# First batch of a fused attention and channel-mixing kernel: ScalarE's DMA issues, weight squares and weight scaling moved to later steps, and value products of two heads put ahead of a score block on TensorE

## The reference

```
q_d, k_d, v_d = means over groups of 4 tokens           # 144 pooled tokens
out_up    = repeat(softmax(q_d k_d^T / 8) v_d, 4)       # pooled attention
out_local = softmax(masked(q k^T / 8)) v                # mask: |i - j| < 4
x   = heads joined: out_up + out_local                  # [4, 576, 512]
u   = x + real(fft over tokens, then over features)
un  = (u - mean) / sqrt(var + 1e-6)
x2  = u + relu(un @ w_ch1) @ w_ch2                      # 512 -> 2048 -> 512
gate = sigmoid(causal convolution of x2 with 5 taps per channel)
out = (gate * (x2 @ w_val)) @ w_out
```

## Time and profile before

| | us |
|---|---|
| median of 3 runs | 789.04 |
| the three runs | 782.66, 790.0, 789.04 |
| the profiled execution, whole | 786.93 |
| its span, first to last instruction | 785.1 |
| TensorE busy | 721.6 (92%) |
| VectorE busy | 387.2 (49%) |
| ScalarE busy | 193.7 (25%) |
| GpSimd busy | 152.2 (19%) |

### The profile page before, as it was taken

The page is one execution under the profiler, slowest core; times in us unless marked ns, Lnnn a source line. Parts: engine busy times, 40 slices in busy tenths (PEclk is TensorE's granted clock), DMA queues, the critical chain, the costliest instruction groups (busy, mean ns, idle before and its releaser), DMA issues.

```text
span 785.1 us, 15614 instructions
## 1 busy us (share of the span) xinstructions
PE 721.6 (92%) x5960; PEld 538.5 (69%) x5960; DVE 387.2 (49%) x925; ACT 193.7 (25%) x417; POOL 152.2 (19%) x130
## 2 busy tenths in 40 slices
PE   2569959999999998999999998999999999999998
PEld 1445547876767776876767776877667677777776
DVE  4447585554535943533544872543553861113452
ACT  1527522222211122322212122222212131111201
POOL 8001777971102221001101311000101300000000
PEclk9999859999999999999999999999999999999999
DMA  9994227032001045022001136022000000000001
GB/s 258 287 247 111 84 91 192 14 72 64 1 1 59 27 130 120 1 65 65 7 1 31 39 85 180 1 58 65 14 1 1 1 31 31 1 1 1 2 15 46
DMA packets 42096, 49.07 MB, mean 62 GB/s; under 512 B 4784, under 2 KB 35568, under 8 KB 40944
## 3 DMA queue, kind: packets, MB, share of 16 engines
q1 hardware_dynamic: 32608, 31.06, 15.7%
q10 hardware_dynamic: 9424, 17.06, 7.0%
HBM read 43.38 MB, written 4.72 MB: 61 GB/s over the span
## 4 chain that ended last, share of the span: by engine, by line
PE 78%; DVE 8%; DMA 5%; issue 3%; POOL 3%; SPq 1%; ACT 1%; ACTq 0%; DVEq 0%; POOLq 0%
PE P L561 23%; PE Y L578 22%; PE P L691 4%; PE Y L680 4%; PE A L587 4%; PE Y L691 4%; DMA kl<-qk_win 3%; DVE prob_or_un L1100 2%; PE A L548 2%; PE A L541 2%; PE A L531 2%; PE A L641 1%; PE A L484 1%; PE A L630 1%; PE P L541 1%
## 5 line engine op out<-in xcount | busy, mean ns | idle before, releaser
L578 PE MATMUL Y<-hT,w 128*128 128x288 f16 x1536 | 215.5, 286 | 5.8 <-DVE xT L1156 5.8
L561 PE MATMUL P<-unT,w_wv 128*128 128x288 f16 x1536 | 212.1, 290 | 6.4 <-issue 5.0
L1135 DVE SCALAR_TENSOR_TENSOR hT<-P,hT 128x288 f16<-128x288 f32 x128 | 58.5, 457 | 268.9 <-ACT hT L815 268.9
L561 PEld LDWEIGHTS P<-unT,w_wv 128*128 128x128 f16 x1536 | 150.1, 99 | 51.7 <-issue 12.0
L578 PEld LDWEIGHTS Y<-hT,w 128*128 128x128 f16 x1536 | 144.9, 98 | 49.8 <-DVE xT L1156 6.1
L815 ACT ACTIVATE hT<-P 128x288 f16<-128x288 f32 x128 | 52.5, 411 | 218.3 <-PE P L561 216.8
L1171 DVE SCALAR_TENSOR_TENSOR gate<-xT,cw,gate 128x288 f32<-128x288 f32 x128 | 68.6, 536 | 4.5
L786 ACT ACTIVATE prob_or_un<-prob_or_un 73x288 f32<-73x288 f32 (+1 forms) x52 | 23.3, 448 | 95.9 <-DVE prob_or_un L1008 92.1
L1306 POOL MEMSET x<- 1x512 f32 x4 | 2.1, 516 | 212.5 <-ACT x L804 212.5
L317 POOL TENSOR_TENSOR x<-x,fb 128x256 f32<-128x256 f32 (+1 forms) x12 | 12.1, 1005 | 107.9 <-DVE fb L1076 107.9
L691 PE MATMUL P<-shared,wo 128*128 128x288 f32 x128 | 32.1, 409 | 0.7 <-DVE shared L1181 0.5
(11 more groups left out here) (162 smaller groups left out, 843.0 us busy)
## 6 DMA issues: line engine op xcount, KB each, us to landing
kl<-qk_win SPq DMA_DIRECT2D x38, 140.0 KB, 5.5
ql<-qk_win SPq DMA_DIRECT2D x19, 256.0 KB, 3.9
vl<-v_win SPq DMA_DIRECT2D x72, 65.0 KB
pair_or_folded<-qk_pool SPq DMA_DIRECT2D x8, 580.0 KB, 5.9
pair_or_spectrum<-qk_pool SPq DMA_DIRECT2D x8, 580.0 KB, 6.5
out<-ot ACTq DMA_DIRECT2D x32, 144.0 KB, 1.8
w_wv<-w_ch ACTq DMA_DIRECT2D x4, 1024.0 KB, 13.3
w<-w_ch ACTq DMA_DIRECT2D x4, 1024.0 KB, 12.6
```

Source lines behind the costliest of these rows:

```text
L561: last = mm(P[s % 2][:, 0:HN], w1s(k, f, wt), unT[:, ut, k, ha * HN:(ha + 1) * HN], start=k == 0 and wt + ut == 0, stop=k == KD - 1 and wt ...
L578: last = mm(Y[d][:, 0:HN], w2s(f, d, wt), hT[s % 3][:, ht, :], start=f == 0 and wt + ht == 0, stop=f == KF - 1 and wt == 1)
L1135: nc.vector.scalar_tensor_tensor(out=hT[s % 3][:, 1, :], in0=P[s % 2][:, 0:HN], scalar=0.0, in1=hT[s % 3][:, 0, :], op0=ALU.max, op1=ALU.s ...
```

## The change

Five tables of the first step get other numbers, `W1_AT` goes from 9 to 10, and on TensorE the scores of local unit 9 move behind the value products of heads 6 and 7. The w1 loads go two steps later, the first two w2 loads one or two, the sixteen issues of the value windows, in groups of four, from steps 2 to 5 to steps 8 to 11, the w1 squares up to two steps later, the w1 halves one step later. The numbers of instructions are the same.

```diff
--- before.py
+++ after.py
@@ -241,13 +241,13 @@
 
         POOLING = {3: 2, 5: 3}
         POOLING_FIRST = {1: 1, 3: 2, 5: 3}
-        WEIGHT_LOADS = {2: [0], 3: [1], 4: [2], 5: [3], 7: [4], 8: [5], 11: [8, 6], 12: [7]}
-        SQUARES = {5: [0, 1], 6: [2, 3], 7: [4, 5], 8: [6, 7], 13: [8], 14: [9, 10], 15: [11], 16: [12, 13]}
-        W1_HIGH = {10: [0, 1], 11: [2, 3], 12: [4], 13: [5], 14: [6], 15: [7]}
-        FIRST_VALUES = {2: (2, 0), 3: (2, 1), 4: (3, 0), 5: (3, 1)}
-        W1_LOW = {11: [0, 1], 12: [2, 3], 13: [4], 14: [5], 15: [6], 16: [7]}
+        WEIGHT_LOADS = {4: [0], 5: [1], 6: [2], 7: [3], 8: [4], 9: [5], 11: [8, 6], 12: [7]}
+        SQUARES = {7: [0, 1], 8: [2, 3, 4, 5], 9: [6, 7], 14: [8, 9], 15: [10], 16: [11, 12, 13]}
+        W1_HIGH = {11: [0, 1], 12: [2, 3], 13: [4, 5], 14: [6], 15: [7]}
+        FIRST_VALUES = {8: (2, 0), 9: (2, 1), 10: (3, 0), 11: (3, 1)}
+        W1_LOW = {12: [0, 1], 13: [2, 3], 14: [4, 5], 15: [6], 16: [7]}
         SEQ_AT, FEAT_AT = 24, 29
-        W1_AT = 9
+        W1_AT = 10
         TILE_ORDER = [0, 3, 1, 4, 2, 5]
         FOLD_AFTER = [2, 3, 4]
         CONSTS = 6 * 16
@@ -706,10 +706,10 @@
                             pair_scores(b, s)
                         elif UD <= s < NU and s != UD + 1:
                             unit_scores(b, s)
-                            if s == UD:
-                                unit_scores(b, s + 1)
                         for u in done:
                             unit_av(b, u)
+                        if s == UD:
+                            unit_scores(b, s + 1)
                 for s in range(SLOTS + LAG_DOWN if m is not None else 0):
                     down = s >= LAG_DOWN
                     if s < SLOTS:
```

## The result

In 20 runs each the changed kernel has a median of 791.49 us (787.3 to 797.09), the kernel before 786.3 (782.66 to 790.19). The ratio is 1.0062, with a 95% interval of 1.0042 to 1.0081: about 4.9 us slower. The forecast was 789.8, within 1% of no change. Its 2.9 us stood against an execution of 786.93, close to the median of the 20 runs, so 2.9 forecast stands against 4.9 measured (3.3 to 6.4 by the interval).

The account below looks back on a forecast made before the run. It took the first batch's attention to be bound by a chain: a key-window DMA, TensorE, then GpSimd. 1.8 at unit 8's transposes plus 1.1 late made 2.9, so 786.93 + 2.9 = 789.8 us, range 783 to 797.

Parts of the forecast that it names:

- Up to head 6, a gain: ScalarE's opening: fewer issues and squares ahead of copies 1 and 3; exponential 6 moves from 33.76 to 31.2.
- Relief of the queues: DMA queues in the opening: without ScalarE's value windows, the second key window lands at 36 to 39 instead of 44.3.
- Copies of heads 5 to 7: ScalarE: value issues at 2.88 a group put copies 5, 6, 7 at 36.1, 43.55, 48.3; copy 7 is 6.4 late.
- The bounds, 1.8 and 5.1 a group: ScalarE's value issues, taken at 2.88 a group: the cheap bound gives 786.6; the dear one adds 6.8 over three groups.
- The swap repairs part of the damage: TensorE, products before unit 9's scores: alone worth up to 3.6; with the issues, unit 8's transposes come 1.8 late.
- The fourth group "takes nothing": ScalarE before unit 8's copy: the fourth value issue ends at worst at 58.4, needed at 58.3; counted as nothing.
- The late stage, +1.1: Step 13 on: second low half and later squares delay unit 11's copy, folds and w2 sum, 1.1 more.
- The sum at the w2 sum: TensorE's w2 sum before the loop: 1.8 + 1.1 = 2.9 us late, at 90.5 instead of 87.58.
- Rival 1: Opening: value issues cost ScalarE next to nothing and TensorE uses the earlier window; 781.7 to 784.4, chance 0.14.
- Rival 2: ScalarE's value issues stall at 5.1 a group, adding 6.8 before copy 7; at least 798.2, chance 0.08.
- The loop unchanged: Channel-mixing loop after about 116 us: shifted by about 3 and otherwise unchanged.

Follow-up runs that it names:

- experiment 3: Changed kernel with the sixteen value issues back in steps 2 to 5, all else changed: 789.36 us, ratio 1.0047 to the kernel before.
- experiment 2: Changed kernel without the swap, scores of unit 9 directly behind those of unit 8 on TensorE: 791.85 us, ratio 1.0041 to the kernel before.
- 6: Kernel before with the TensorE swap and W1_AT 10 instead of 9, tables as before: 790.01 us, ratio 1.0017.
- experiment 4: Changed kernel with one w1 high and one low half a step from step 13 on, instead of two: 790.01 us, ratio 1.0051 to the kernel before.
- experiment 5: Kernel before with only the changed late stage (w1 halves, and squares from step 14 on): 789.74 us, ratio 1.0012.
- experiment 7: Kernel before with the swap, W1_AT 10, DFT tables one step later and the w2 loads behind them two steps later: 785.89 us, ratio 0.9961.
- experiment 8: Kernel before with swap, W1_AT 11, changed w1 loads, later tables, single halves, value issues in ScalarE's gaps: 786.72 us, ratio 0.9988.
- experiment 9: Changed kernel with value issues back in steps 2 to 5, single w1 halves, later DFT tables and w2 loads: 784.15 us, ratio 0.9952 to kernel before.
- experiment 10: Changed kernel with only the DFT tables and the w2 loads behind them later: 791.54 us, ratio 1.0058 to the kernel before.
- experiment 1: Kernel before with only the TensorE swap (products of heads 6 and 7 ahead of unit 9's scores): 790.24 us, ratio 1.0051.

## Why the prediction was right, point by point

The range, the sign and the class held; the sum was 2 us short, just outside the measured interval of 3.3 to 6.4. The range, 783 to 797, took in a gain as well as a loss, so that it held says little; the milestones say more. Taking the trace of after against the steps:

- **Up to head 6, a gain**: right. Exponential 6 at 30.74 (31.2 forecast).
- **Relief of the queues**: the direction was right, the size too small. I put the key window of unit 9 at 36 to 39; its two DMAs were issued from 13.17 on and took about 11 to 13 us, so it landed near 26. "They trade packet for packet" held, 505 to 508 and 99 to 95 now, and so did the end of the first w1 loads at about 22. What I left out is the stretch behind it: with almost nothing on ScalarE's queue SyncE's moved 943 packets in 3 us, against 508 in 7 before.
- **Copies of heads 5 to 7**: the step right, its term too small. 36.30 (36.1 forecast), 44.53 (43.55) and 49.71 (48.3). The groups of four issues took 3.46, 3.41 and 3.23 us from first to last (32.26 to 35.72 is the first), not the 2.88 of the earlier trace rows. The excess, 0.58 + 0.53 + 0.35 = 1.5, is about the miss at unit 8's transposes: +3.2 instead of +1.8. The trace of the kernel before already had such a group, its first, which I did not take:

```profile
8.25 3.47 ACTq L875 DMA_DIRECT2D unT<-v_win  x4
```

The bounds, 1.8 and 5.1 a group, took it in. This is **the largest mis-sized term of the sum**, with the clock below. Experiment 3 shows the cause: with the issues back, the transposes come at 49.0.
- **The swap repairs part of the damage**: wrong, though the sum it stands in held (from unit 9's scores to unit 8's transposes 4.1 us, 51.20 to 55.27, against 7.6 before). Without the swap unit 9's scores were not late at all (40.88 in experiment 2). Experiments 2 and 6 show that with the later scale it is worth 3.6 where TensorE waits for the window of unit 9, and that it costs 0.9 where head 7's copy is late.
- **The fourth group "takes nothing"**: off by 0.6 (+3.8 at unit 8's product, +3.2 at its transposes). I had counted the 2.86 of the value issues, not the three issues of step 11 behind them, ahead of the same copy: two of tables, 0.45 and 0.47 (56.82, 57.30), and a w2 load that took 1.73 (57.80) instead of the 0.38 of the earlier trace rows.
- **The late stage, +1.1**: the mechanism is in the trace: two low halves make the fold late, TensorE stood 1.08 for it (0.25 with single halves, experiment 4). Its price in time is not shown: experiment 5 has +0.9 for this part alone, with an interval from -0.6 to +2.4. Nor are two halves the only thing that makes this wait: experiments 7 and 8, with single ones, waited 1.47 and 0.82. What I had not in the sum is TensorE's level. The 2.54 us for unit 11's copy only used up what two units at the upper level had won (unit 10's transposes at 68.42 against 64.64, +3.8; unit 11's product at 77.39 against 73.65, +3.7). But after it the level was the lower one, granted 0.50 from 78 to 90, and the first twelve matmuls of the DFT took 2.29 + 2.30 + 2.08 instead of what the kernel before shows:

```profile
80.29 3.96 PE L587 MATMUL A<-sdft,pair_or_folded 128*128 128x289 f32 x8
84.18 1.33 PE L587 MATMUL P<-sdft,pair_or_folded 128*1 128x289 f32 x4
```

6.67 against 5.29 is 1.4 us. From unit 12's product (+3.7) to the w2 sum (+6.2) the loss is 2.5 = 1.08 + 1.4. That the stand of 2.54 brought the lower level is not shown: the same twelve took 6.3, 6.5 and 6.3 us in experiments 3, 8 and 9, which had neither that stand nor an upper stretch before it, and 4.8 in experiment 5. So the kernel before may have been fast by chance here; why the level rises sooner in one trace than in another is open.
- **The sum at the w2 sum**: 2.9 + 1.4 (issues) + 0.6 (fourth group) + 1.4 (level) = 6.3; the trace has 6.2. Over many runs it is 4.9; both traces are of single executions, in which the place of the upper level and of the late window varies.
- **Rival 1 (relief)**: its premise, cheap issues, is refuted: 2.9 to 3.5 us a group. (The estimate of 0.2 a group, worked out from the 50 ns of dispatch in the Trainium skill, DMA: Bandwidth & Descriptors, Anatomy of one DMA, does not hold here; that section describes DMAs issued by GpSimd, not by ScalarE.) But experiment 8 went where the rival would have gone, with transposes at 43.8, and even there the time was only that of the kernel before: the rival left out that the next window would be late.
- **Rival 2 (stall at 5.1 a group)**: didn't come; the groups stayed at 3.5 or under.
- **The loop unchanged**: right. From the mixing start to the end it is 668.9 us before and 668.4 now.

What the runs show of the whole: the early issues cost the changed kernel about 6 us at unit 8 (experiment 3), and the traffic around 50 us decides whether an earlier TensorE keeps them (7 against 6, which differ only in `WEIGHT_LOADS`: 1.0017 to 0.9961; 9 against 3: 1.0047 to 0.9952). The runs show no gain for either alone (3 and 10). Open: how much of experiment 9's gain over 3 and 10 the single low halves bring, since 4 alone moved the ratio by 0.001; and why the place of TensorE's upper level varies.

## What to carry to other kernels

A DMA issue on a compute engine is an instruction of that engine: place it where the engine waits anyway (experiment 8's sixteen held up no copy), and count all issues ahead of the copy that somebody needs. When a wait is removed, ask which transfer is wanted next and what runs beside it: here the gain came only when 2.2 MB of loads that nobody needed for 20 us and more were moved out of the way. One trace tells the mechanism, the ratio of many runs tells the worth; where they disagree, look first where the traced execution lies among the runs (787.08 against a median of 791.54 in experiment 10), then at the clock's stretches.

## What was not expected of the hardware

- The issues have no one price: half a value window, in four issues, took 3.47 us and then 2.88 in the kernel before, 2.86 to 3.46 in the changed kernel, and a single w2 load of 1 MB 0.38 to 1.73.
- The granted clock in the rows doesn't tell TensorE's level before its first fall. Of the changed kernel, columns: stretch, its length, TensorE's busy time (matmuls), granted clock, DMA share, GB/s:

```profile
60.00:64.00 4.00, 3.74 (x57) 1.00 0.99 384
...
78.00:82.00 4.00, 4.00 (x32) 0.50 0.02 4
```

In both stretches the four transposes of a unit took 1.07 us (62.12 and 79.12), the duration of the lower level, 1.2 GHz; at the upper one, 2.4 GHz, they took 0.63 (73.35). The durations tell the level, the 1.00 doesn't.
- In the traces with an upper stretch among the units it ended during or just after a stand of TensorE: 5.17 us for a window in experiment 1, 2.54 for ScalarE in the changed kernel and experiment 2, 1.56 in experiments 4 and 10, 0.70 in experiment 7. Where it never came in the local units and they ran without a stand (experiment 9), the DFT also began at the lower level (4.62 us for the eight matmuls that took 3.96 before).
